# Order of the ScalarE and VectorE work in the recurrences, one turned group in another bank, and z ahead of the portions, in a fused gated-attention kernel

## The chip, the core and the metric

The kernel runs on one core of a Trainium2 chip. The metric is device microseconds of one execution, the median over runs. The kernel before takes 607.09 us (median of three runs, 606.45 to 607.91). The engines have short names: PE is TensorE, DVE is VectorE, ACT is ScalarE, POOL is GpSimd, SP is SyncE, which here only issues transfers.

## The reference

Three stages follow each other, for 4 batches of 768 tokens and 384 features, all in float32.

1. Gated linear attention, 8 heads of 48: `state = sigmoid(f) * state + k v`, `y = q state`, token by token.
2. A mixture of 4 attention experts of width 64: `softmax(scale * q k^T, causal) v wo` per expert, of which each token takes the two with the highest gate logits, weighted by their softmax.
3. `theta = x @ w_theta; z = (x cos theta, x sin theta); y = w_tok_r zr + w_tok_i zi; u = x + y; out = u + relu(u @ w_ch)`. The token mixing is a product of 768x768 with 768x384, twice a batch.

## The kernel before, in words

The tokens of a batch are cut into six chunks (or tiles) of 128, the heads into four pairs. Products that need float32 accuracy are made of three products of halves: a rounded part (`_h`, written by ACT) and the rest (`_l`, written by DVE, or by POOL for weights). Every engine has one queue, worked off in the order in which the code writes it, and the engines wait for each other by counting semaphores. So a line that waits also holds whatever is written behind it. `it` is the batch.

**Gates.** The gate logits of a batch go through five steps, in place in the tile `gate`: DVE clamps (`clamp_gates`, L804), ACT takes exp (`exp_gates`, L502) and ln(1+x) (`log_gates`, L507), DVE sums along the tokens (`scan`, L808), ACT writes exp(-sum) to `next_decay` together with a copy of the chunk sums (`shrink_pair`, L525) and exp(sum) in place (`grow_pair`, L531). POOL multiplies q by the first and k by the second (`scale`, L432). In batch 0 this goes by three parts of the tokens (`shrink_first`, `grow_first`, `scan_first`, `scale_first_q`, `scale_first_k`), with DVE scaling; in the others by pair, during the batch before. SP may load the gates of pair p of batch b+1 only when k of pair p of batch b is scaled (L346), since both use the same part of `gate`. `worst_sum` (DVE) takes the largest chunk sum and `worst_over_rows` (POOL, an all-reduce over the partitions) the largest over the rows; the flag `steep` that DVE makes of it decides on a slow path that the data never take, and DVE and ACT read it from memory at the end of each recurrence.

**Recurrence** (six chunks). PE makes masked scores, turns k (`turn_k`, L1223), adds the increments of the state and the outputs; DVE masks the scores (L935) and carries the state (L951, L955); ACT copies the turned k (`kTs`, L636) and the outputs (`xn`, L639). The code of the gates of the next batch is written between these.

**Ring.** PE turns xn to xT (L1382), then makes V with the gate logits of the experts (`wvg`) and q and k of the experts (`wqk`) through a ring of banks. DVE copies V, computes the routing (L1019 to L1039) and writes `qk_l` (L1058); ACT writes `xT_h` (L700) and `qk_h` (L704).

**Jobs.** Six jobs j of expert attention: scores (L1299), maxima on DVE (L1049), exp on ACT (L677), transposes of the probabilities in groups of at most four tiles (L1327), their copies (L1069 DVE, L713 ACT), the product with V into bank 7 (L1354). The turned groups use banks 4, 5 and 6 in turn: group g waits until group g-3 is copied. Every second job, `portions` (DVE, L1075 to L1079) makes the weight of each token for each expert, PE turns it (L1337), ACT copies it (L721) and DVE multiplies (`weigh_outputs`, L1091). At job 7 DVE clamps the gates of batch it+2, and PE begins the next batch's scores.

**Weights.** ACT and POOL split `wo`, its product with `w_theta` and `w_ch` into halves in the jobs of batch 0. The token weights are split in the jobs of batch 3 and later.

**Mixing.** Per batch six z tiles (`z_hi`, `z_lo`) times the token weights (`mix`), then the channel product. It begins inside the last jobs of batch 3, at job 6.

Of the kernel before, what the change touches and what calls it, by code (L numbers as in the profile page):

```python
# [22 lines left out]
P = 128  # L23
# [11 lines left out]
PART = 4  # L35
# [81 lines left out]
NG = len(GROUPS)  # L117

# [56 lines left out]
def build(nc, fT, qT, kT, vT, v, wq, wk, wv, w_gate, wo, woT, w_theta, w_tok, w_ch, out):  # L175
    with ExitStack() as ctx:
# [80 lines left out]
        worst_of_all = s1("worst_of_all", [P, 1])  # L257
        steep = s1("steep", [P, 1], I32)
# [146 lines left out]
        def _(pool):  # L405
# [41 lines left out]

            worst_over_rows(0)
# [33 lines left out]
            for tile in range(2 * TOKENS_FIRST):  # L482
                if tile >= 2 and tile % 2 == 0:
                    pool.wait_ge(spread_done, upto(B - 1, len(TILES), tile // 2))
                token_weights(tile)
# [15 lines left out]
        def _(act):  # L501
# [67 lines left out]

            def split_outputs(b):  # L570

                nc.scalar.copy(OT_h[:, :, :], OT[:, b:b + 1, :].rearrange("p b (a t) -> p (b a) t", a=2)).then_inc(oh, 1)
# [55 lines left out]
            for it in range(B):  # L628

                def recurrence_copies():  # L630
                    for c in range(NT):
                        if c < NT - 1:
# [3 lines left out]
                            nc.scalar.copy(kTs[:, c % 2, :], ps(7)).then_inc(kt_copied, 1)  # L636
                        if c >= 1:
                            act.wait_ge(y_done, upto(it, NT, c))
                            nc.scalar.copy(xn[:, c - 1, :], ps(4 + (c - 1) % 2)[:, 0:D]).then_inc(x_copied, 1)  # L639
                        if it < 1:  # L640
                            if c == 1:
                                shrink_first(2)
                                grow_first(2)
                            elif c == 3:
# [5 lines left out]
                            elif c in (4, 5):  # L650
                                exp_gates(it + 1, range(2 * c - 8, 2 * c - 6))
                        elif it < B - 1:
                            if c in (0, 1):
                                log_gates(it + 1, range(2 * c, 2 * c + 2))
# [25 lines left out]
                for n in [*range(RING_X), *range(FIRST_QK, RING)]:  # L680
                    if n == FIRST_QK:
# [7 lines left out]
                        if it < 1:  # L689
                            log_gates(it + 1)  # L690
                        if it < B - 1:
                            grow(it + 1, 0)
                            grow(it + 1, 1)
# [15 lines left out]
                def copy_turned(m):  # L709
                    for r in range(2):  # L710
                        g = group(m, r, PART)
                        act.wait_ge(pt_done, upto(it, NG, g + 1))
                        nc.scalar.copy(probT[:, m % 2, r, PART * P:WIDE], ps(4 + g % 3)[:, 0:WIDE - PART * P]  # L713
                                       ).then_inc(pt_copied[1], 1)

                def copy_portion(tp):
# [4 lines left out]
                    nc.scalar.copy(portion[:, :, :, :].rearrange("p w a t -> p (w a t)"), ps(4 + g % 3)  # L721
                                   ).then_inc(pt_copied[1], 1)

                for j in range(JOBS + 2):
# [8 lines left out]
                    if it < B - 1:  # L733
                        if j == (3 if it < 1 else 1):
                            shrink_pair(it + 1, 3)
                        elif j == (4 if it < 1 else 2):
                            grow_pair(it + 1, 3)
                    if it < 1:
                        if j == 1:
                            shrink_pair(1, 2)  # L740
                        elif j == 2:
                            grow_pair(1, 2)
                        elif j == 5:
                            act.wait_ge(w_in[2], 16)
                            hi(wx_h[:, :, 0:D], staged(W_O, 768, 2), w_hi)
                        elif j == 6:
                            hi(wx_h[:, :, D:2 * D], staged(W_OTH, 768, 2), w_hi)
                        elif j == 7:
                            act.wait_ge(w_in[4], 16)
                            hi(wch_h[:, :, :], staged(W_CH, 1152), w_hi)  # L750
                    if j == JOBS + 1 and it < B - 2:
                        exp_gates(it + 2)
                    if it > B - 2:
                        if j < 2 * TOKENS_FIRST:
                            token_weights(j)
                        if j == JOBS + 1:
                            split_outputs(0)

# [35 lines left out]
        def _(dve):  # L794
# [134 lines left out]
            for it in range(B):  # L929
# [11 lines left out]
                for c in range(NT - 1):  # L941
# [17 lines left out]
                    if it < 1:  # L959
# [559 lines left out]
```

## Time and profile before

| | |
|---|---|
| median of the runs | 607.09 us |
| the profiled execution | 607.17 us |
| its span, first to last instruction | 605.5 us |
| PE busy | 565.9 us, 93% |
| DVE, ACT, POOL busy | 377.0, 300.8, 128.0 us |
| recurrence, ring, jobs of batch 1 | 108 to 128, 128 to 155, 155 to 187 us |
| mixing, four batches | from 352 us on |
| mean granted PE clock | 0.997 of full speed |

Times in the rows are from the start of the span. A row of a timeline gives start, busy time, engine, line, operation, what it writes and reads, the count, and in brackets the idle time of that engine just before with what ended it. "issue" is time for which the profile shows no releaser.

### The profile page before, as it was taken

What the parts mean: (1) busy time and instruction counts of PE and PEld (TensorE: products, weight loads), DVE (VectorE), ACT (ScalarE), POOL (GpSimd) and SP (SyncE); (2) the same over time, 40 slices, a digit from 0 to 9 for tenths busy, and PEclk for the clock granted to TensorE, in tenths of its full rate; (3) what the DMA queues carried; (4) which work ended last, traced back from release to release, by engine and by line L of the source; (5) the groups of instructions that cost most, each with busy time, mean ns of one, the idle gap of its engine ahead of it and who ended that gap; (6) DMA issues with size and microseconds to landing.
All of it is one profiled execution on the core that took longest, in us unless ns stands there. A gap on an engine that the chain in (4) does not pass through costs nothing.

```text
span 605.5 us, 13205 instructions
## 1 busy us (share of the span) xinstructions
PE 565.9 (93%) x5532; PEld 522.5 (86%) x5532; DVE 377.0 (62%) x695; ACT 300.8 (50%) x623; POOL 128.0 (21%) x87
## 2 busy tenths in 40 slices
PE   0979899989999999999999989999999999999997
PEld 0779788889778897889997779999999999999997
DVE  3977877768677687766477748756244533454324
ACT  5658577644767356743377727513341334124311
POOL 1003431402330004400023216602220132013110
PEclk9999999999999999999999989999999999999999
DMA  8938111043110070000710000001000100010002
GB/s 289 318 108 289 37 44 28 2 160 130 54 54 2 15 276 1 1 1 4 260 55 2 1 1 2 0 15 66 0 1 1 70 9 1 1 53 28 0 1 79
DMA packets 17966, 37.19 MB, mean 61 GB/s; under 512 B 2160, under 2 KB 10608, under 8 KB 17392
## 3 DMA queue, kind: packets, MB, share of 16 engines
q1 hardware_dynamic: 17904, 36.32, 17.3%
q8 instruction: 44, 0.72, 0.5%
q14 instruction: 18, 0.15, 0.1%
HBM read 31.46 MB, written 4.72 MB: 60 GB/s over the span
## 4 chain that ended last, share of the span: by engine, by line
PE 75%; DVE 11%; ACT 9%; issue 3%; DMA 1%; SPq 0%; DVEq 0%; ACTq 0%
PE bank L1162 17%; PE bank L1163 16%; PE bank L1164 16%; PE bank L1327 5%; PE bank L1299 5%; PE bank L1354 4%; ACT prob L677 3%; PE bank L1180 3%; DVE nmax L1049 3%; PE bank L1260 2%; PE bank L1256 2%; PE bank L1444 1%; PE bank L1241 1%; PE bank L1227 1%; DMA gate<-fT 1%
## 5 line engine op out<-in xcount | busy, mean ns | idle before, releaser
L1162 PE MATMUL bank<-z_h,wt_h 128*128 128x384 f32 x288 | 98.3, 341 | 1.8 <-DVE z_l L889 1.8
L1163 PE MATMUL bank<-z_l,wt_h 128*128 128x384 f32 x288 | 98.1, 340 | 0.0
L1164 PE MATMUL bank<-z_h,wt_l 128*128 128x384 f32 x288 | 97.2, 338 | 0.0
L677 ACT ACTIVATE prob<-bank,nmax 128x384 f32<-128x384 f32 (+5 forms) x96 | 59.9, 630 | 26.9 <-DVE nmax L1049 26.7
L1049 DVE TENSOR_REDUCE nmax<-bank 128x1 f32<-128x384 f32 (+5 forms) x96 | 55.0, 618 | 20.9 <-PE bank L1305 14.6
L496 POOL TENSOR_TENSOR trig<-trig,x 128x768 f32<-128x768 f32 x18 | 33.6, 1865 | 151.9 <-ACT trig L597 92.6
L904 DVE TENSOR_SCALAR turns<-bank 128x384 int32<-128x384 f32 x22 | 12.2, 556 | 72.9 <-PE bank L1164 72.9
L1162 PEld LDWEIGHTS bank<-z_h,wt_h 128*128 128x128 f32 x288 | 54.4, 189 | 2.5 <-issue 2.2
L1163 PEld LDWEIGHTS bank<-z_l,wt_h 128*128 128x128 f32 x288 | 54.6, 189 | 0.0
L1164 PEld LDWEIGHTS bank<-z_h,wt_l 128*128 128x128 f32 x288 | 54.5, 189 | 0.0
L780 ACT CAST uT_h<-bank 128x384 fp32r<-128x384 f32 x24 | 11.5, 478 | 81.0 <-PE bank L1444 81.0
L1327 PE MATMUL bank<-ident,prob 128*128 128x128 f32 x336 | 46.0, 279 | 5.7 <-ACT portion L721 3.2
L1327 PEld LDWEIGHTS bank<-ident,prob 128*128 128x128 f32 x336 | 36.2, 141 | 14.1 <-ACT portion L721 5.1
L1354 PE MATMUL bank<-probT,Vm 128*64 128x128 f32 x672 | 42.0, 276 | 0.0
L1354 PEld LDWEIGHTS bank<-probT,Vm 128*64 128x64 f32 x672 | 36.2, 137 | 4.0 <-issue 4.0
L935 DVE TENSOR_TENSOR probT<-bank,keep 128x1024 f32<-128x1024 f32 x24 | 29.0, 1218 | 13.9 <-PE bank L1180 12.4
L589 ACT COPY x<-bank 128x384 f32<-128x384 f32 x24 | 11.6, 481 | 49.7 <-PE bank L1164 44.8
L1260 PE MATMUL bank<-V,probT 128*64 128x48 f32 x768 | 35.8, 219 | 0.0
L1162 PE MATMUL bank<-xT_h,wqk_h 128*128 128x384 f32 x96 | 32.9, 343 | 0.0
L1260 PEld LDWEIGHTS bank<-V,probT 128*64 128x64 f32 x768 | 31.9, 138 | 0.7 <-DVE probT L935 0.5
L1163 PE MATMUL bank<-xT_l,wqk_h 128*128 128x384 f32 x96 | 32.4, 338 | 0.0
L1164 PE MATMUL bank<-xT_h,wqk_l 128*128 128x384 f32 x96 | 32.4, 337 | 0.0
(177 smaller groups left out, 1391.8 us busy)
## 6 DMA issues: line engine op xcount, KB each, us to landing
V<-v SPq DMA_DIRECT2D x4, 1152.0 KB, 10.0
gate<-fT SPq DMA_DIRECT2D x12, 384.0 KB, 3.1
q<-qT SPq DMA_DIRECT2D x12, 384.0 KB, 6.1
k<-kT SPq DMA_DIRECT2D x12, 384.0 KB, 6.6
wt_raw<-w_tok SPq DMA_DIRECT2D x6, 768.0 KB, 8.0
out<-x SPq DMA_DIRECT2D x24, 192.0 KB, 1.9
gate<-fT SPq DMA_DIRECT2D x3, 512.0 KB, 4.9
q<-qT SPq DMA_DIRECT2D x3, 512.0 KB, 10.3
```

The lines of the kernel that those rows point to most:

```text
L496: nc.gpsimd.tensor_tensor(trig[:, s % 2, :, :], trig[:, s % 2, :, :], x2[:, s:s + 1, :].broadcast_to([P, 2, D]), ALU.mult).then_inc(z_made, 1)
L677: nc.scalar.activation(prob[:, m % 2, r, at], bank[r][:, at], ACT.Exp, bias=nmax[:, m, k:k + 1], accum_out=den[:, m // 2, which, e:e + 1]) ...
L935: nc.vector.tensor_tensor(Am[:, c % 2, :, :], bank[c % 2][:, :].rearrange("p (h t) -> p h t", h=H), keep[:, None, :].broadcast_to([P, H, P ...
L1049: nc.vector.tensor_reduce(nmax[:, m, k:k + 1], bank[r][:, columns_of(m, which)], X, ALU.max, negate=True).then_inc(max_done, 1)
L1162: nc.tensor.matmul(o, a_h, b_h, start=start, stop=False)
L1163: nc.tensor.matmul(o, a_h, b_l, start=False, stop=False)
L1164: return nc.tensor.matmul(o, a_l, b_h, start=False, stop=stop)
L1180: mm = nc.tensor.matmul(bank[c % 2][:, slot(h):slot(h) + P], k[r:r + 64, h // 2, at], q[r:r + 64, h // 2, at], start=True, stop=True)
L1260: mm = nc.tensor.matmul(ps(4 + c % 2)[own, h * HD:(h + 1) * HD], Am[:, c % 2, slot(h) // P, own], V[:, c, h * HD:(h + 1) * HD], start=(c = ...
L1299: mm = nc.tensor.matmul(bank[r][:, lo_:hi_], x[rows, a, queries], y[rows, 2 + a, keys], start=fresh_bank and n == 0, stop=False, skip_grou ...
L1327: mm = nc.tensor.transpose(ps(4 + g % 3)[:, (c - n) * P:(c - n + 1) * P], prob[:, m % 2, r, c * P:(c + 1) * P], ident[:, :])
L1354: mm = nc.tensor.matmul(ps(7)[64 * r:64 * r + 64, at], Vm[:, s, e * ED:(e + 1) * ED], probT[:, m % 2, r, n * P:(n + 1) * P], start=s == 0, ...
```

## The change

In the recurrences: in batch 0, ACT's growths of part 2 move behind the kTs copy of chunk 2, DVE scales k of part 2 right after q, and the clamps and exponentials of the next batch's gates move to chunk 4 and 5 and behind the ring's xT. In batches 1 and 2, ACT takes one pair's logarithm in each of the first four chunks, and the growth of pair 0 moves from the ring into chunks 4 and 5. In the jobs of batch 0, ACT shrinks or grows one pair in every job; the late weights move to the ring of batch 1. DVE's scan of pair 3 in batch 0 moves behind the maxima of job 0. POOL runs one all-reduce at its start, of which nothing uses the result. Turned group 3 goes to bank 7. In batch 3, DVE writes z_l of tile 0 in front of the portions of job 6, and token weight 5 moves to job 7.

```diff
+def turn_bank(g):
+    return 7 if g == 3 else 4 + g % 3
...
@@ gpsimd
+            nc.gpsimd.partition_all_reduce(warm[:, :], halfpi[:, :], P, bass.bass_isa.ReduceOp.max).then_inc(consts, 1)
             worst_over_rows(0)
...
             for tile in range(2 * TOKENS_FIRST):
+                if tile == 2 * TOKENS_FIRST - 1:
+                    pool.wait_ge(ol, 2)
                 token_weights(tile)
@@ scalar
+            def late_weights():
+                act.wait_ge(w_in[2], 16)
+                act.wait_ge(w_in[4], 16)
+                act.wait_ge(wth_copied, 1)
+                hi(wx_h[:, :, 0:D], staged(W_O, 768, 2), w_hi)
+                hi(wx_h[:, :, D:2 * D], staged(W_OTH, 768, 2), w_hi)
+                hi(wch_h[:, :, :], staged(W_CH, 1152), w_hi)
...  recurrence_copies, for c in range(NT), behind the copy to kTs
+                        if it < 1 and c == 2:
+                            shrink_first(2)
+                            grow_first(2)
...  behind the copy to xn
-                            if c == 1:
-                                shrink_first(2)
-                                grow_first(2)
-                            elif c in (4, 5):
-                                exp_gates(it + 1, range(2 * c - 8, 2 * c - 6))
+                            elif c == NT - 1:
+                                exp_gates(1, (0, 1))
                         elif it < B - 1:
-                            if c in (0, 1):
-                                log_gates(it + 1, range(2 * c, 2 * c + 2))
+                            if c < PAIRS:
+                                log_gates(it + 1, range(c, c + 1))
+                            elif c == NT - 2:
+                                shrink_pair(it + 1, 0)
+                            else:
+                                grow_pair(it + 1, 0)
...  ring, n == FIRST_QK
                         if it < 1:
-                            log_gates(it + 1)
-                        if it < B - 1:
-                            grow(it + 1, 0)
+                            exp_gates(1, (2, 3))
+                            log_gates(1)
+                            grow(1, 0)
+                        elif it < B - 1:
+                            if it == 1:
+                                late_weights()
                             grow(it + 1, 1)
...  jobs
-                    if it < B - 1:
-                        if j == (3 if it < 1 else 1):
-                            shrink_pair(it + 1, 3)
-                        elif j == (4 if it < 1 else 2):
-                            grow_pair(it + 1, 3)
-                    if it < 1:
-                        (j 1, 2: shrink_pair(1, 2), grow_pair(1, 2); j 5, 6, 7: hi of wx_h, wx_h, wch_h)
+                    if it < 1 and 1 <= j <= JOBS:
+                        (shrink_pair if j % 2 == 1 else grow_pair)(1, (j + 1) // 2)
+                    elif 1 <= it < B - 1 and j == 1:
+                        shrink_pair(it + 1, 3)
+                    elif 1 <= it < B - 1 and j == 2:
+                        grow_pair(it + 1, 3)
                     if it > B - 2:
-                        if j < 2 * TOKENS_FIRST:
+                        if j < 2 * TOKENS_FIRST - 1:
                             token_weights(j)
                         if j == JOBS + 1:
                             split_outputs(0)
+                            token_weights(2 * TOKENS_FIRST - 1)
@@ vector
...  recurrence of batch 0, behind the state of chunk c
                         elif c == 1:
                             scale_first_q(2)
                             worst_sum(0)
-                        elif c == 2:
                             scale_first_k(2)
-                        elif c in (3, 4):
-                            clamp_gates(1, 2 * c - 6)
-                            clamp_gates(1, 2 * c - 5)
+                        elif c == NT - 2:
+                            clamp_gates(1, 0)
+                            clamp_gates(1, 1)
...  behind the last xT_l
+                if it < 1:
+                    clamp_gates(1, 2)
+                    clamp_gates(1, 3)
...  ring, behind qk_l of tile n (in batch 0 both scans stood here, at n 1 and 3)
                     if n == FIRST_JOB:
                         row_max(0)
+                        if it < 1:
+                            scan(1, 3)
...
+                    if it < 1 and n == 1:
+                        scan(1, 2)
+                    elif 1 <= it < B - 1 and n == 3:
+                        scan(it + 1, 3)
...  jobs
-                    if j == 4 and it < B - 1:
+                    if j == (JOBS if it < 1 else 4) and it < B - 1:
                         worst_sum(it + 1)
...
+                    if it > B - 2 and j == JOBS:
+                        z_lo(0, 0)
                     if j >= 2 and j % 2 == 0:
                         portions((j - 2) // 2)
-                        if j == JOBS:
-                            z_lo(0, 0)
@@ tensor, turn_probs (ps(4 + g % 3) is ps(turn_bank(g)) here and in all copies)
-                        if g >= 3:
-                            pe.wait_ge(pt_copied[turned_by(g - 3)], copies(it, g - 3))
+                        if g >= 4:
+                            before = g - 3 if g != 6 else 0
+                            pe.wait_ge(pt_copied[turned_by(before)], copies(it, before))
...  weigh_values
+                    if m < 1:
+                        pe.wait_ge(pt_copied[turned_by(3)], copies(it, 3))
```

## Rows read from the trace of the kernel before

**Rows 1.** The page, busy time and share of the span, PE.

```profile
PE 565.9 (93%) x5532; PEld 522.5 (86%) x5532; DVE 377.0 (62%) x695; ACT 300.8 (50%) x623; POOL 128.0 (21%) x87
```
**Rows 2.** Waits of PE by line: total us, times, longest.

```profile
PE bank L1227 <- ACT kTs L636: 2.7, 3, 1.0
...
PE bank L1327 <- DVE probT L1069: 2.5, 4, 0.6
```
**Rows 3.** Timeline of PE in the recurrence of batch 0.

```profile
31.52 0.66 PE L1227 MATMUL bank<-ident,k 128*128 128x128 f32 x4 [0.91 <-ACT kTs L636]
...
35.31 1.16 PE L1180 MATMUL bank<-q,k 64*128 64x128 f32 x16 [0.94 <-DVE k L833]
...
43.92 0.39 PE L1256 MATMUL bank<-S,q 128*64 128x96 f32 x4 [1.37 <-issue]
```
**Rows 4.** Timeline of DVE there.

```profile
41.53 1.22 DVE L935 TENSOR_TENSOR probT<-bank,keep 128x1024 f32<-128x1024 f32 x1 [1.55 <-issue]
```
**Rows 5.** Timeline of POOL there and in the ring.

```profile
37.50 0.38 POOL L429 PARTITION_ALL_REDUCE worst_of_all<-worst  x1 [33.33 <-issue]
...
46.34 1.82 POOL L446 TENSOR_TENSOR wvg_l<-prob,wvg_h 128x768 fp32r<-128x768 f32 x1 [8.47 <-issue]
...
48.30 3.51 POOL L446 TENSOR_TENSOR wqk_l<-OT,wqk_h 128x1536 fp32r<-128x1536 f32 x1
```
**Rows 6.** DVE and PE in the ring of batch 0, and DVE's clamps by line.

```profile
46.95 2.88 DVE L889 TENSOR_TENSOR xT_l<-bank,xT_h 128x384 fp32r<-128x384 f32 x6 [2.07 <-ACT xT_h L700]
...
53.49 1.75 DVE L812 TENSOR_TENSOR_SCAN gate<-fresh,gate 128x768 f32<-128x768 f32 x1
...
71.98 0.50 PE L1299 MATMUL bank<-qk_h 64*128 64x512 f32 x2 [1.07 <-DVE qk_l L1058]
...
L806 DVE TENSOR_SCALAR gate<-gate,floor 128x768 f32<-128x768 f32 x12 | 6.7, 613 | 0.0
```
**Rows 7.** End of batch 0: ACT, POOL, the gates' transfer, DVE, PE.

```profile
102.91 0.84 ACT L568 CAST wx_h<-OT 128x768 fp32r<-128x768 f32 x1
...
94.05 1.81 POOL L443 TENSOR_TENSOR k<-k,gate 128x768 f32<-128x768 f32 x1 [3.50 <-ACT gate L534]
...
gate<-fT SPq DMA_DIRECT2D x12, 384.0 KB, 3.1
...
105.52 0.76 DVE L1091 TENSOR_TENSOR OT<-bank,portion 128x256 f32<-128x256 f32 x2 [1.49 <-PE bank L1354]
...
106.88 0.66 PE L1227 MATMUL bank<-ident,k 128*128 128x128 f32 x4
```
**Rows 8.** Timelines of ACT and PE in batch 1's recurrence.

```profile
108.83 1.28 ACT L510 ACT_TABLE_LOAD   x1
...
110.13 1.58 ACT L510 ACTIVATE gate<-gate 128x768 f32<-128x768 f32 x2
...
112.23 0.66 PE L1227 MATMUL bank<-ident,k 128*128 128x128 f32 x4 [1.01 <-ACT kTs L636]
```
**Rows 9.** PE ahead of the fifth xT tile in batches 1 and 3.

```profile
131.10 1.01 PE L1382 MATMUL bank<-ident,xn 128*128 128x128 f32 x6 [1.49 <-DVE xT_l L889]
...
294.61 1.01 PE L1382 MATMUL bank<-ident,xn 128*128 128x128 f32 x6 [0.18 <-DVE xT_l L889]
```
**Rows 10.** DVE, POOL and PE at job 6 of batch 3, and granted clock by window.

```profile
348.64 1.55 DVE L1075 TENSOR_SCALAR share<-den 128x8 f32<-128x8 f32 x1
...
348.33 1.82 POOL L470 TENSOR_TENSOR wt_l<-wt_raw,wt_h 128x768 fp32r<-128x768 f32 x1 [4.51 <-ACT wt_h L584]
...
352.16 0.41 PE L1162 MATMUL bank<-z_h,wt_h 128*128 128x384 f32 x1 [1.82 <-DVE z_l L889]
...
355.88 0.60 PE L1337 MATMUL bank<-ident,spread 128*128 128x128 f32 x4
...
350.00:354.00 4.00, 2.18 (x10) 1.97 (x9) 1.95 (x4) 0.48 (x1) 0.16 (x1) 0.81 0.00 0
...
366.00:370.00 4.00, 4.00 (x25) 4.00 (x24) 2.75 (x4) 3.97 (x7) 1.55 (x1) 1.00 0.00 0
```

More of the change, by code:

```diff
@@ L257, in build @@
         worst_of_all = s1("worst_of_all", [P, 1])
+        warm = s1("warm", [P, 1])
         steep = s1("steep", [P, 1], I32)
@@ L640, in recurrence_copies @@
                         if it < 1:
-                            if c == 1:
-                                shrink_first(2)
-                                grow_first(2)
-                            elif c == 3:
+                            if c == 3:
                                 act.wait_ge(w_in[0], 32)
@@ L712, in copy_turned @@
                         act.wait_ge(pt_done, upto(it, NG, g + 1))
-                        nc.scalar.copy(probT[:, m % 2, r, PART * P:WIDE], ps(4 + g % 3)[:, 0:WIDE - PART * P]
+                        nc.scalar.copy(probT[:, m % 2, r, PART * P:WIDE], ps(turn_bank(g))[:, 0:WIDE - PART * P]
                                        ).then_inc(pt_copied[1], 1)
@@ L720, in copy_portion @@
                         act.wait_ge(ot_done, upto(it, NT, NT + 2 * tp))
-                    nc.scalar.copy(portion[:, :, :, :].rearrange("p w a t -> p (w a t)"), ps(4 + g % 3)
+                    nc.scalar.copy(portion[:, :, :, :].rearrange("p w a t -> p (w a t)"), ps(turn_bank(g))
                                    ).then_inc(pt_copied[1], 1)
@@ L732, in _ @@
                         copy_turned(j - 1)
-                    if it < B - 1:
-                        if j == (3 if it < 1 else 1):
-                            shrink_pair(it + 1, 3)
-                        elif j == (4 if it < 1 else 2):
-                            grow_pair(it + 1, 3)
-                    if it < 1:
[L739 to L750, printed above, removed]
+                    if it < 1 and 1 <= j <= JOBS:
[4 more added lines that the diff above has]
+                        grow_pair(it + 1, 3)
                     if j == JOBS + 1 and it < B - 2:
@@ L1061, in _ @@
                                                    op1=ALU.subtract).then_inc(ring_free, 1)
-                    for p, last in ((2, 1), (3, 3)) if it < 1 else ((3, 3),):
-                        if n == last and it < B - 1:
-                            scan(it + 1, p)
+                    if it < 1 and n == 1:
+                        scan(1, 2)
+                    elif 1 <= it < B - 1 and n == 3:
+                        scan(it + 1, 3)
                 def copy_turned(m, r):
@@ L1068, in copy_turned @@
                     dve.wait_ge(pt_done, upto(it, NG, g + 1))
-                    nc.vector.tensor_copy(probT[:, m % 2, r, 0:PART * P], ps(4 + g % 3)).then_inc(pt_copied[0], 1)
+                    nc.vector.tensor_copy(probT[:, m % 2, r, 0:PART * P], ps(turn_bank(g))).then_inc(pt_copied[0], 1)
                 def portions(tp):
@@ L1112, in _ @@
                     if it > B - 2:
-                        if j == JOBS:
-                            z_lo(0, 0)
-                        elif j == JOBS + 1:
+                        if j == JOBS + 1:
                             split_outputs(0)
@@ L1323, in turn_probs @@
                         g = group(m, r, n)
-                        if g >= 3:
-                            pe.wait_ge(pt_copied[turned_by(g - 3)], copies(it, g - 3))
+                        if g >= 4:
+                            before = g - 3 if g != 6 else 0
+                            pe.wait_ge(pt_copied[turned_by(before)], copies(it, before))
                         for c in range(n, min(n + PART, KEYS)):
-                            mm = nc.tensor.transpose(ps(4 + g % 3)[:, (c - n) * P:(c - n + 1) * P],
+                            mm = nc.tensor.transpose(ps(turn_bank(g))[:, (c - n) * P:(c - n + 1) * P],
                                                      prob[:, m % 2, r, c * P:(c + 1) * P], ident[:, :])
@@ L1332, in turn_portions @@
                     g = group(2 * tp + 1, None, 0)
+                    assert g > 6
                     pe.wait_ge(spread_done, upto(it, len(TILES), tp + 1))
@@ L1336, in turn_portions @@
                         for a in range(2):
-                            mm = nc.tensor.transpose(ps(4 + g % 3)[:, (2 * w + a) * P:(2 * w + a + 1) * P],
+                            mm = nc.tensor.transpose(ps(turn_bank(g))[:, (2 * w + a) * P:(2 * w + a + 1) * P],
                                                      spread[:, w, 2 * a:2 * a + 2, :], ident[:, :])
```

## The prediction

> **What bounds the kernel now.** I read four views in this order. The busy times: TensorE (PE) is busy 566 of 605.5 us [rows 1], so a change can pay only where PE stands idle or runs slowly. PE's waits by line: apart from the first weights' arrival, which is not touched, the idle time is small change, repeated per batch: a stall before the transposes of xT (step 7), 2.7 us on copies of kTs, 2.5 us before the fourth turned group of the first job [rows 2]. Then the timelines of each engine around every such stall, and last the granted clock, which is 1.00 everywhere but from 352 to 356 us.
>
> **Method.** I replay each changed stretch with the durations of the rows and say how much earlier (minus) or later (plus) PE passes a point than before. Times are in the frame of the kernel before; what comes earlier in the program shifts both sides alike. A stall taken off PE counts in full only if the next thing PE needs is ready; I name that thing each time.
>
> **1. Recurrence of batch 0: -2.4 us.** PE waits three times: 0.91 us for the copy kTs of chunk 2, which stands on ScalarE (ACT) behind the growths of part 2; 0.94 us for k scaled by VectorE (DVE); 1.37 us for the last state [rows 3]. The new order puts the kTs copy ahead of the growths: turn_k(3) goes to 30.6. k is scaled right after q, from 31.8 to 33.0, instead of 33.95: scores(4) start at 33.4, when outputs(2) end. DVE loses two clamps (1.1 us) ahead of reading the steep flag, so S of chunk 3 is there at 37.5, the flag is written at 37.6, its read takes 1.55 us [rows 4], the last mask (1.22 us) runs from 39.1, Su and S follow by 41.4. PE starts outputs(5) at 41.5, not 43.92. What is late next is that same chain: PE still idles some 0.7 us there. What can eat this gain is GpSimd (POOL): V's tiles need wvg_l, which is ready at 48.3, just as PE got there [rows 5]. Its start at 46.34 came 8.5 us after the all-reduce, which itself was recorded 5.7 us after its input (31.78). If these gaps are fixed after the time the all-reduce is asked for, nothing moves and the gain is 0.1. The added all-reduce runs at about 4 us, when POOL is free, and nothing else of POOL stands between it and the real one: I take it that the real one then comes at 32, the next operation is possible from 40.5, and wvg_l starts with the state of chunk 4, at 41.5. Range -2.5 to -0.1.
> The Trainium skill (GPSIMD Engine Reference, Instruction dispatch) says that the first call of a freshly loaded POOL kernel pays about 6 us of code load; the gap of 5.7 us agrees. By it the warm call moves this load to the start of the program.
>
> **2. Ring of batch 0: -0.5 us.** Two clamps (0.61 us, 0.55 apart) now stand behind the last xT_l (end 49.83) and ahead of the copies of V. The exponentials of pairs 2 and 3 (1.58 us as a pair, like the logarithms) follow, then the table load of 1.28 us, so the first logarithm is there at 54.15 and scan 0 starts at 54.2 instead of 53.49 [rows 6, 8]: the routing and the first four qk_l are 0.65 late, and so are the first scores. But scan 3 (1.75 us) now stands behind the maxima of the first job, no longer ahead of them. These are 0.9 earlier, the exponentials of job 0 too, qk_l of the last tile ends at 71.4, and the piece of PE that waited for it starts at 71.5 instead of 71.98. ACT drops one pair's growth there (1.6 us) for the two exponentials. Upper bound +1.5: a clamp that meets wqk_l (3.5 us on POOL [rows 5]) waits for its end, and by the old times of POOL, less 2.4 us only in what is in front, that costs DVE 2 us. That such waits exist is shown by a tensor_scalar of 8 elements that took 1.55 us and ended with POOL's wt_l [rows 10]. By the times that I take, wqk_l ends at 47.0 and the clamp begins at 47.4.
> The skill (SBUF — State Buffer, Who interferes with whom) has it that a VectorE tensor_scalar in a 2-port mode and GpSimd block each other for a whole instruction; the trace agrees (those 1.55 us). By this rule the ring is -0.5 or +1.5, according to the 0.4 us between the two times.
>
> **3. Fourth turned group in bank 7: 4 x -0.6 = -2.4 us.** It no longer waits for DVE's copy of group 0; the rows have 2.5 us in four times [rows 2]. Next needed is exp_done of job 1 (75.2 against 74.8 plus a piece of scores), then the maxima of job 2, for which DVE waited on PE anyway. Bank 7 was last read before job 1's scores, and the values that use it wait for this group's copy, a whole job later. Range -1.2 to -2.5: ACT's growth of 0.85 us just behind can hold half of it.
>
> **4. End of batch 0: +3.9 us.** This is the step that speaks against the change. Pair 3's growth moves from job 4 to job 6, behind the copy that ends at 102.95, where wx_h stood [rows 7]. So gate grows by 103.75 and POOL scales k of pair 3 (1.81 us) until 105.6; before, it started that at 94.05. SyncE loads the gates of pair 3 of batch 2 only after it: 3.1 us to landing, 108.75. DVE clamps them in front of the last weighing of outputs, in the same queue: clamp until 109.35, the two products (0.76) until 110.1; before, they started at 105.52. PE needs these for turn_k(0) of batch 1: 110.15 instead of 106.88. DVE's first mask (1.22) then ends at 111.3, and outputs(0), which followed turn_k at 107.47, starts at 111.3: +3.9. Bounds: 0 (the transfer lands before 105) and +5.5 (POOL and DVE collide in scaling and clamps: twice 0.8).
>
> **5. Clock after that idle: +0.8 us.** PE idles 3.3 us there. After the idle of 1.82 us at 352 the granted clock of the next 4 us was 0.81 [rows 10], and work of 2.1 us took 3.7. Between nothing (after 1.49 us at 131 it stayed 1.00) and those 1.6 I take the middle, as DVE sets the pace of that stretch.
>
> **6. Waits for kTs: -2.0 us.** The table load of 1.28 and two logarithms (1.58) stand between two kTs copies in batches 1 and 2; PE waited 1.01 [rows 8] and 0.8 (2.7 in three [rows 2], less 0.91 and 1.01). With one logarithm the copy is 0.75 earlier: -0.7 in batch 2. In batch 1 ACT works on while PE stands still (step 4), so both waits, 0.3 for the first copy and 1.01, go: -1.3. The other logarithms stand where ACT idles 1.2 to 2.8 us a chunk.
>
> **7. Table load ahead of xT_h: 2 x -1.2 = -2.4 us.** In batches 1 and 2, where the last function ahead of the branch is the logarithm, 1.28 us of load stand at L700 and PE waits 1.49; in batch 3, without it, 0.18 [rows 9]. Now a growth comes ahead of the branch; its own load and exponential (2.3 us) lie in chunk 4, behind the copy of chunk 3 and well ahead of that of chunk 4. ACT's late weights of batch 1 (2.85 us) take the place of a growth of 1.7 and the idle time before the scan; POOL's parts of them are done 25 us before they are needed. Worst case -1.0 for both (another load stays), best -2.6.
>
> **8. z_l in front of the portions: -3.5 us.** z_l waited behind share, reciprocal and spread, 2.4 us with the collision of [rows 10]; token weight 5, which caused it, is moved too. z_l now ends at 349.5, PE's transposes end at 350.3, and mix starts then, not at 352.16: -1.85. Spread (until 350.7) is ready before mix ends. Without the idle the clock stays up, and the twelve products that took 3.7 us (352.16 to 355.88) take 2.1, at the pace of 25 in 4 us after 366: -1.6. Range -1.8 to -3.5.
>
> **Sum.** -2.4 - 0.5 - 2.4 + 3.9 + 0.8 - 2.0 - 2.4 - 3.5 = -8.5 us. The profiled execution took 607.17 us in all (span 605.5), the median of three is 607.09, so they are one number: 607.2 - 8.5 = 598.7 us.
>
> **Rivals.**
> A, the gates of batch 2 are not late: landing by 105.5, or clamped after the weighing. For: 3.1 us is a median. Against: the order on every queue. Steps 4 and 5 go and step 6 shrinks to -1.7: 594.3 us.
> B, POOL is as late as before: wvg_l starts near 46.3, PE waits for it, and the clamps of step 2 run into wqk_l: -0.1 and +1.5 for -2.4 and -0.5, together 603.0 us.
> C, slower: the clock stays low. One mechanism, at the start of batch 1: after 3.3 us without PE work the clock falls, and the small products of the recurrence do not raise it. At 0.81 the products of [rows 10] took 1.76 times as long, so 1 us of old work costs 0.76 more. It has to hold for 11 us of work to eat 8.5 us; over the whole recurrence and ring of batch 1 (46 us) it would cost up to 35. With the 20 us until the next dense stretch it gives 613 us. Against: at 352 it was back after 4 us.
> D, the small gains do not add (3 and 7 are taken back by ACT in the same job or ring): half of 3, 6 and 7, so +3.4: 602.1 us.
>
> **Chances.** Forecast 0.52, A 0.14, B 0.14, D 0.14, C 0.06. All but C are faster by more than 0.2% (1.2 us, about what a measurement of this kernel can tell); I leave 0.04 for no change where B and D come together with the collisions of step 4. So faster 0.90, same 0.04, slower 0.06. Range: A below and B above belong in it, 594.0 to 603.5; C is left out.
>
> **What would show it.** Step 1: outputs(5) of batch 0 starts 2.4 us earlier and wvg_l's gap is gone. Step 2: the first clamp behind xT_l takes 0.6 us, or over 2. Step 3: no wait at L1327 for DVE's probT. Step 4: between the batches DVE idles some 4 us before a clamp that waits for gate's DMA, and PE waits about 3.3 us at the first turn_k of batch 1. Step 5: PEclk under 1 there. Step 7: no table load at L700. Step 8: no wait of PE for z_l, PEclk 1.00 near 350. If step 4 doesn't show, the time is near 594; if the clock is low for more than 10 us in batch 1, the sign is wrong.

## The result

The changed kernel takes 601.34 us (median of four runs, 598.96 to 602.51) against 607.5 us of the kernel before in the same rounds. The medians differ by 6.2 us. The ratio is 0.9895, with a 95% interval of 0.9857 to 0.9933, which by itself gives 6.4 us less, between 4.1 and 8.7. The forecast was 8.5 less. The profiled execution is the slowest of the four, 602.51 us with a span of 600.8 and a mean granted clock of 0.991 (before: 0.997); the fastest had 0.996. The clock is thus one part of the spread.

The waits of PE by line, in the profile after (total us, times, longest):

```profile
PE bank L1320 <- DVE qk_l L1078: 3.2, 5, 1.9
...
PE bank L1248 <- DVE OT L1112: 3.1, 1, 3.1
...
PE bank L1349 <- ACT portion L748: 3.0, 8, 0.4
...
PE bank L1277 <- issue: 1.4, 4, 0.7
...
PE bank L1407 <- DVE xT_l L905: 0.9, 4, 0.4
...
PE bank L1360 <- DVE spread L1100: 0.3, 1, 0.3
```

The waits of [rows 2] for kTs and for probT are gone, the one for xT_l (3.6 us before) is down to 0.9. Two are new or grown: 1.88 us for qk_l in the ring of batch 0 and 3.05 us for OT at the end of batch 0. The next fences follow these two through the engines. First the ring of batch 0, timelines of POOL, DVE and PE and the granted clock (the number before the last two of a window's row):

```profile
14.12 0.41 POOL L456 PARTITION_ALL_REDUCE warm<-halfpi  x1 [9.95 <-issue]
...
32.96 1.13 POOL L437 PARTITION_ALL_REDUCE worst_of_all<-worst  x1 [18.42 <-DVE worst L854]
...
43.97 1.82 POOL L454 TENSOR_TENSOR wvg_l<-prob,wvg_h 128x768 fp32r<-128x768 f32 x1 [9.88 <-issue]
...
45.93 3.50 POOL L454 TENSOR_TENSOR wqk_l<-OT,wqk_h 128x1536 fp32r<-128x1536 f32 x1
```
```profile
48.09 2.29 DVE L822 TENSOR_SCALAR gate<-gate,floor 128x768 f32<-128x768 f32 x2
...
53.65 1.76 DVE L828 TENSOR_TENSOR_SCAN gate<-fresh,gate 128x768 f32<-128x768 f32 x1 [1.74 <-ACT gate L521]
```
```profile
65.02 0.59 PE L1320 MATMUL bank<-qk_h 64*128 64x384 f32 x2 [1.88 <-DVE qk_l L1078]
```
```profile
65.20:68.50 3.30, 3.30 (x21) 2.19 (x22) 2.06 (x5) 1.23 (x4) 0.00 (x0) 0.50 0.00 0
```

POOL's wqk_l is in flight from 45.93 to 49.43. DVE's two clamps need 1.15 us elsewhere and 2.29 here: the first one waits for POOL. Scan 0, which in [rows 6] came without a wait, waits 1.74 us for the logarithm behind them, PE waits 1.88 us for the first scores, and then works at half its clock until 68.5.

Then the end of batch 0, timelines of ACT, POOL, DVE and PE, and the clock:

```profile
102.86 0.85 ACT L545 ACTIVATE gate<-gate 128x768 f32<-128x768 f32 x1
```
```profile
103.85 2.25 POOL L451 TENSOR_TENSOR k<-k,gate 128x768 f32<-128x768 f32 x1 [1.48 <-ACT gate L545]
```
```profile
101.05 1.34 DVE L1096 TENSOR_SCALAR share<-den 128x8 f32<-128x8 f32 x1
...
109.25 0.62 DVE L822 TENSOR_SCALAR gate<-gate,floor 128x768 f32<-128x768 f32 x1 [2.74 <-DMA gate<-fT]
...
109.78 0.75 DVE L1112 TENSOR_TENSOR OT<-bank,portion 128x256 f32<-128x256 f32 x2
```
```profile
110.68 1.09 PE L1248 MATMUL bank<-ident,k 128*128 128x128 f32 x4 [3.05 <-DVE OT L1112]
```
```profile
109.60:116.30 6.70, 5.62 (x63) 4.88 (x64) 3.75 (x6) 4.25 (x6) 0.38 (x1) 0.50 0.01 2
```

This is the chain of step 4 link by link: growth of pair 3 until 103.7, POOL's scaling until 106.1, the transfer, DVE idle 2.74 us "<-DMA gate<-fT", the clamp, the products, and PE after 3.05 us of nothing. The scaling took 2.25 us in place of 1.81, beside DVE's other clamps. The clock is 0.50 from 109.6 to 116.3, and PE works for 5.6 us of that. In [rows 7] DVE began the same products at 105.52 and PE its transposes at 106.88 without a wait.

Last, three places where the change gained: the last state of the first recurrence, the xT transposes of batch 1, and z_l:

```profile
42.25 0.39 PE L1277 MATMUL bank<-S,q 128*64 128x96 f32 x4 [0.73 <-issue]
```
```profile
134.54 1.01 PE L1407 MATMUL bank<-ident,xn 128*128 128x128 f32 x6 [0.18 <-DVE xT_l L905]
```
```profile
347.57 0.95 DVE L905 TENSOR_TENSOR z_l<-x,z_h 128x768 fp32r<-128x768 f32 x1
...
348.43 0.16 DVE L1096 TENSOR_SCALAR share<-den 128x8 f32<-128x8 f32 x1
```

The wait of 1.37 [rows 3] is 0.73, that of 1.49 [rows 9] is 0.18. z_l ends at 348.5, share behind it takes 0.16 us instead of 1.55 [rows 10], and PE shows no wait for z_l and a clock of 1.00 there.

How far PE is ahead of (-) or behind (+) the kernel before at the start of the same work, and what each stretch gave against its step:

| PE starts | before | after | difference | stretch | forecast |
|---|---|---|---|---|---|
| first scores, batch 0 | 20.89 | 21.84 | +0.95 | +0.95 (start) | 0 |
| xT of batch 0 | 45.65 | 43.98 | -1.67 | -2.62 (step 1) | -2.4 |
| first turned group, batch 0 | 73.01 | 73.91 | +0.90 | +2.57 (step 2) | -0.5 |
| scores of job 2, batch 0 | 75.54 | 75.58 | +0.04 | -0.86 (step 3) | -0.6 |
| outputs(0) of batch 1 | 107.47 | 111.71 | +4.24 | +4.20 (step 4) | +3.9 |
| turn_k(2) of batch 1 | 112.23 | 116.98 | +4.75 | +0.51 (steps 5, 6) | -0.5 |
| V of batch 1 | 132.03 | 135.47 | +3.44 | -1.31 (step 7) | -1.2 |
| scores of job 2, batch 1 | 158.11 | 160.72 | +2.61 | -0.83 (step 3) | -0.6 |
| turn_k(2) of batch 2 | 194.00 | 195.92 | +1.92 | -0.69 (step 6) | -0.7 |
| V of batch 2 | 213.81 | 214.40 | +0.59 | -1.33 (step 7) | -1.2 |
| scores of job 2, batches 2 and 3 | 323.51 | 322.44 | -1.07 | -1.66 (step 3) | -1.2 |
| portions of job 7, batch 3 | 355.88 | 351.21 | -4.67 | -3.60 (step 8) | -3.5 |

### The profile page after: what moved, and what is told of

Its sections match the earlier page's. It is cut to its first block, busy times and chain, and to the rows that moved or that the text cites. A ratio compares the mean times of both kernels' runs of the same rounds, so it can differ in the third digit from the quotient of the medians.

```text
span 600.8 us, 13212 instructions
## 1 busy us (share of the span) xinstructions
PE 568.6 (95%) x5532; PEld 524.8 (87%) x5532; DVE 379.5 (63%) x695; ACT 300.7 (50%) x623; POOL 131.5 (22%) x88
## 4 chain that ended last, share of the span: by engine, by line
PE 81%; DVE 8%; ACT 6%; DMA 2%; issue 2%; SPq 1%; POOL 0%; DVEq 0%; ACTq 0%; POOLq 0%
PE bank L1183 17%; PE bank L1184 16%; PE bank L1185 16%; PE bank L1349 6%; PE bank L1320 5%; PE bank L1379 4%; PE bank L1201 3%; ACT prob L701 3%; PE bank L1281 3%; PE bank L1277 2%; PE bank L1248 2%; PE bank L1262 2%; DVE nmax L1067 2%; PE bank L1469 1%; DMA OT<-w_theta 1%
```

## The experiments

**1. Growths of batch 1's pairs in the order of before.** The version called early_growth:

```diff
                             log_gates(1)
                             grow(1, 0)
+                            grow(1, 1)
...
-                    if it < 1 and 1 <= j <= JOBS:
-                        (shrink_pair if j % 2 == 1 else grow_pair)(1, (j + 1) // 2)
+                    if it < 1 and 1 <= j <= 4:
+                        (shrink_pair if j % 2 == 1 else grow_pair)(1, (j + 1) // 2 + 1)
...
-                    if j == (JOBS if it < 1 else 4) and it < B - 1:
+                    if j == 4 and it < B - 1:
```

> The changed kernel with the growths of batch 1's pairs in the order of before: pairs 0 and 1 in the ring, pair 2 in jobs 1 and 2, pair 3 in jobs 3 and 4 (and the worst sum at job 4). Theory: the late growth of pair 3 delays the gates of batch 2, DVE's clamp and PE. Then PE's wait of 3.05 us at the first turn_k of batch 1, its wait of 0.3 for spread and the low clock behind (about 1.5) go, and about 1 us of the waits for kTs comes back less than before: 3.9 us less than the changed kernel's 601.3, so 597.4 us. Rival: PE's wait there has another cause (the chain of the last values), it stays, and the time is 601 within the noise. Second rival: the growth back in the ring delays the routing's exponential and the first scores by 1 us or more: above 598.5.

594.23 us (593.46 to 595.23), ratio to the kernel before 0.9792 (0.976 to 0.9823): 7.1 less than the changed kernel. The wait for OT is gone, and so is every wait for kTs. Between the portions of job 7 and turn_k(2) of batch 1, PE gains 5.8 us on the changed kernel (from -2.74 to -8.55): 3.05 of wait, 0.3 in the scores ahead of it (1.95 us in the changed kernel, whose last k POOL had ready at 106.1, and 1.61 here), and 2.3 in work that ran at half clock. This end of batch 0 cost more than steps 4 and 5 said, because I had put 0.8 us on the low clock. The other 2.7 us by which the two profiles differ are the start (1.1; PE's first scores at 20.75, not 21.84), 0.3 at the portions, and 1.4 in the ring, where a wait of 2.00 us is not followed by a low clock here. So of the 7.1 us between the medians some 6 belong to the edit, and the rest is what differs from one execution to the next.

**2. All four clamps in chunk 4 of the recurrence.** The version early_clamps:

```diff
                         elif c == NT - 2:
-                            clamp_gates(1, 0)
-                            clamp_gates(1, 1)
+                            for p in range(PAIRS):
+                                clamp_gates(1, p)
...
-                if it < 1:
-                    clamp_gates(1, 2)
-                    clamp_gates(1, 3)
```

> The changed kernel with all four clamps of batch 1's gates in chunk 4 of batch 0's recurrence, none behind the last xT_l. Theory: the clamp behind xT_l waits for POOL's wqk_l, and with what follows makes PE wait 1.9 us for the first scores, after which its clock falls. DVE has 2 us idle behind chunk 4's clamps, so nothing else moves: the clamps end before xT_l begins, scan 0 starts about 1.5 us earlier, PE's wait of 1.9 us shrinks under 0.4 and the clock stays up in the ring: 3.1 us less than 601.3, so 598.2 us. Rival: the exponentials of pairs 2 and 3 on ACT with the table load set the start of scan 0, not the clamp: the wait stays over 1 us and the time is over 600.

598.9 us (597.69 to 599.43), ratio 0.9859 (0.9829 to 0.989); 2.4 less than the changed kernel. Its wait of 1.88 us is gone, the four waits of PE for qk_l are 1.3 us in all, and scan 0 starts without one. DVE's clamps now meet POOL's wvg_l, and take 3.79 us instead of 2.2; PE pays 0.5 for that (0.9 us of wait for xT_l in place of 0.4):

```profile
PE bank L1317 <- DVE qk_l L1075: 1.3, 4, 0.3
...
PE bank L1245 <- DVE OT L1109: 3.1, 1, 3.1
```
```profile
40.66 3.79 DVE L822 TENSOR_SCALAR gate<-gate,floor 128x768 f32<-128x768 f32 x4
```

**3. Both edits together,** version both.

> Both of these edits. Theory: they are independent (one is paid in the ring, one at the end of batch 0), so 3.9 and 3.1 add: 594.3 us. Rival: the second growth in the ring on ACT takes back 1 us of it: 595.3 us or more.

592.81 us (592.5 to 594.06), ratio 0.9764 (0.9735 to 0.9793). It is 8.5 us below the changed kernel and 14.7 below the kernel before. The second edit is worth only 1.4 on top of the first, not 3.1: by the profiles it gains 1.9 in the ring and loses 0.5 ahead of it, at the wait for xT_l, and early_growth had no low clock in the ring that could go.

**4. What holds the clamp: POOL makes wqk_l later.** On early_growth:

```diff
+            pool.wait_ge(clamped, gates(1, PAIRS))
             lo(wqk_l[:, :, :], staged(W_QK, 1536), wqk_h[:, :, :], wqk_lo)
```

> The early_growth version (594.2 us), in which POOL makes wqk_l only when the clamp of pair 3 of batch 1 is done. In early_growth the two clamps behind the last xT_l took 2.10 us, in recurrence 1.14, and PE waited 2.0 us for the first scores. Theory: the 0.95 us more is the wait for wqk_l, in flight on POOL. Then the two clamps take 1.15 us, scan 0 starts 0.95 earlier, PE's wait falls to about 1.0 (two clamps, two exponentials and the table load remain ahead of scan 0), and wqk_l is done before q and k need it: 593.3 us. Rival: the clamps were slow for another reason: they stay at 2.1 and the time at 594.2 or more.

593.08 us (592.76 to 593.61), ratio 0.9773 (0.9756 to 0.9789). The clamps and PE's wait, in early_growth and then here:

```profile
46.99 2.10 DVE L823 TENSOR_SCALAR gate<-gate,floor 128x768 f32<-128x768 f32 x2
```
```profile
64.04 0.44 PE L1321 MATMUL bank<-qk_h 64*128 64x384 f32 x2 [2.00 <-DVE qk_l L1079]
```
```profile
47.05 1.14 DVE L824 TENSOR_SCALAR gate<-gate,floor 128x768 f32<-128x768 f32 x2
```
```profile
63.15 0.44 PE L1322 MATMUL bank<-qk_h 64*128 64x384 f32 x2 [1.04 <-DVE qk_l L1080]
```

2.10 us became 1.14, and 2.00 became 1.04: the clamp did wait for wqk_l, and PE paid all of it. The other 1.0 us of wait is the late clamps' own work with the exponentials and the table load, of which step 2 had 0.6.

**5. When POOL can go on.** On both, POOL waits for the state of chunk 3 instead of chunk 4 ahead of wvg_l (`pool.wait_ge(s_ready, NT - 2)`), version pool_early:

> Both edits, and POOL waits for the state of chunk 3, not of chunk 4, ahead of wvg_l. In the changed kernel the all-reduce was recorded until 34.1, the state of chunk 4 was there at 42.15 and wvg_l started at 43.97. Theory 1 (the gap is fixed after the all-reduce, 8.5 to 9.9 us): wvg_l starts at 42.6 to 44.0 as now. Theory 2 (a start about 2 us after the wait is met): the state of chunk 3 is there at 38.3, wvg_l starts near 40.2. In time: 594.3 us in either case by my account, as PE gets to V when wvg_l is ready either way; by theory 2 POOL's reads may slow DVE's last states, up to 1 us more.

592.72 us (592.1 to 592.95), ratio 0.9762 (0.9732 to 0.9791), level with both. Timelines of POOL, pool_early first, then both:

```profile
32.05 1.13 POOL L437 PARTITION_ALL_REDUCE worst_of_all<-worst  x1 [16.25 <-DVE worst L855]
...
42.37 2.17 POOL L454 TENSOR_TENSOR wvg_l<-prob,wvg_h 128x768 fp32r<-128x768 f32 x1 [9.19 <-issue]
```
```profile
33.31 1.13 POOL L437 PARTITION_ALL_REDUCE worst_of_all<-worst  x1 [17.96 <-DVE worst L855]
...
43.95 1.83 POOL L454 TENSOR_TENSOR wvg_l<-prob,wvg_h 128x768 fp32r<-128x768 f32 x1 [9.51 <-issue]
```

The operation starts 9.2 us after the all-reduce's end here and 9.5 there, though the wait was met a chunk (some 4 us) earlier; by theory 2 it would have started near 40. So most of the gap hangs on the all-reduce, not on the wait. In all versions with the added all-reduce it is 9.2 to 9.9.

**6. Without the all-reduce at the start,** version no_warm, on both:

> The same version (592.8 us) without the all-reduce at the start. Theory: the first all-reduce that runs carries about 6 us of code load, wherever it is. Then the real one is recorded 5.7 us or more behind its input, not 0.35, and what POOL does next comes about 9.5 us after it: wvg_l starts near 48, not 43.9, PE waits 2 us or more for it ahead of V, and the flag is read up to 1 us later: 595 to 597 us. Rival: the gap behind the all-reduce counts from when it was asked for, as in the kernel before (8.5 us after its record, 14.2 after its input): wvg_l starts near 46.5, and the cost is under 1 us: 593.5 us.

```profile
37.40 0.38 POOL L437 PARTITION_ALL_REDUCE worst_of_all<-worst  x1 [33.23 <-issue]
...
44.56 1.82 POOL L454 TENSOR_TENSOR wvg_l<-prob,wvg_h 128x768 fp32r<-128x768 f32 x1 [6.78 <-issue]
```
```profile
37.81 0.15 DVE L994 TENSOR_SCALAR steep<-worst_of_all 128x1 int32<-128x1 f32 x1 [0.77 <-POOL worst_of_all L437]
```

593.85 us (593.05 to 595.95), ratio 0.9794 (0.977 to 0.9818), 1.0 more than both; the intervals overlap, but the profile shows the mechanism. The all-reduce is recorded 5.9 us behind its input (31.5, not shown) instead of 0.2, DVE waits 0.77 us for it, and PE's longest wait at L1275 grows from 0.7 to 1.6. But POOL goes on after 6.8 us instead of 9.5. The rival was right: the added all-reduce takes 5.7 us away ahead of the real one, and 2.7 come back behind it. From its first scores to its first product for V, PE takes 0.6 us longer than in both, so that is what the added all-reduce is worth here.

The theory was wrong in a second point: the 6 us are not a cost of the first all-reduce alone. In the profiles of all versions, every `worst_over_rows` that comes behind other work of POOL, in batches 1 to 3 too, is recorded 5.7 to 6.6 us after its input and that work were done.

**7. Group 3 back in bank 4,** version bank3, on both (`return 4 + g % 3`, and its wait for group 0):

> The version with early growth and early clamps (592.8 us), with group 3 turned into bank 4 again, as before the change. Theory: PE waits 0.63 us for DVE's copy in each of the four batches, and only that comes back: 2.5 us more, 595.3 us. Rival: the waits come back but the next one (for ACT or DVE in the same job) shrinks by as much: 592.8 to 593.8 us.

596.12 us (595.87 to 600.36), ratio 0.9842 (0.9803 to 0.9881), 3.3 more. PE's four waits for probT return with 2.5 us. From the first turned group to the scores of job 2 it takes 2.53 us again, as in the kernel before, and not 1.68; of the 0.85 us next to nothing comes back in the same job, so 0.8 us a batch is lost. The waits of the products and of the weight loads (PEld):

```profile
PE bank L1346 <- DVE probT L1088: 2.5, 4, 0.6
```
```profile
PEld bank L1346 <- DVE probT L1088: 3.5, 4, 0.9
```

The weight loads, which run ahead of the products, stood still for the whole 3.3 to 3.5 us; the rows on the products alone, which I had used, show less.

**8. z_l and token weight 5,** on both. z_half puts z_lo behind the portions again; z_old also puts token weight 5 back to job 5 and takes POOL's wait for ol away.

> The same version (592.8 us) with z_l of tile 0 behind the portions again, but token weight 5 still at job 7. Theory: z_l then waits for share, reciprocal and spread without a collision with POOL, 1.05 us, and PE, which was 0.7 us behind z_l, waits about 0.4 us; the clock stays up: 593.2 us. Rival: the order alone was the cause of the old wait of 1.82 us: 596 us.

> The same version (592.8 us) with z_l behind the portions and token weight 5 at job 5, both as before the change. Theory: share waits for POOL's wt_l (1.55 us in place of 0.16), PE waits 1.8 us for z_l and its clock falls for about 3 us of work, which costs 1.6 more: 596.3 us. Rival: without the fall of the clock 594.6 us.

z_half 593.3 us (592.42 to 593.71; ratio 0.9769, 0.9752 to 0.9785), z_old 595.78 (594.61 to 596.15; ratio 0.9808, 0.9792 to 0.9824). Timelines of PE and DVE, z_half and then z_old, and z_old's clock behind the wait:

```profile
340.21 0.41 PE L1181 MATMUL bank<-z_h,wt_h 128*128 128x384 f32 x1 [0.44 <-DVE z_l L906]
```
```profile
342.61 0.41 PE L1178 MATMUL bank<-z_h,wt_h 128*128 128x384 f32 x1 [1.82 <-DVE z_l L903]
```
```profile
339.09 1.55 DVE L1091 TENSOR_SCALAR share<-den 128x8 f32<-128x8 f32 x1
```
```profile
342.60:346.60 4.00, 3.99 (x40) 3.79 (x42) 0.00 (x0) 1.18 (x2) 0.00 (x0) 1.00 0.01 4
```

Of the old wait of 1.82 us, 0.44 comes from the order alone and 1.4 from share waiting for POOL. The two together cost 3.0 us in the median, 2.1 in the profiles. The clock did not fall in z_old's profile.

**9. The clamp of pair 3 out of the way,** on the changed kernel, version late_clamp:

```diff
-                            for p in range(PAIRS):
+                            for p in range(PAIRS - (it < 1)):
                                 clamp_gates(it + 2, p)
...  behind mask(0)
+                elif it == 1:
+                    clamp_gates(2, 3)
...  ACT, job 7, and chunk 0 of batch 1
-                        exp_gates(it + 2)
+                        exp_gates(it + 2, range(PAIRS - (it < 1)))
+                            if it == 1 and c == 0:
+                                exp_gates(2, (3,))
```

> The changed kernel (601.3 us) with one move at the end of batch 0: the clamp of pair 3 of batch 2's gates stands behind the first mask of batch 1 on DVE, its exponential behind the first copy of kTs on ACT; the late growths stay. Theory: what stops PE is that the clamp, which waits for the transfer, stands in front of the last weighing of outputs. Then PE's wait of 3.05 us at turn_k(0) goes, although the gates land at the same time; a wait of 1.5 to 2 us for kTs of chunk 1 comes, as ACT waits for the clamp and then loads its table; the clock may still fall: 597.5 to 600 us. Rival: POOL's late scaling of k is what delays PE (the scores of heads 6 and 7 wait for it): then the wait stays 3 us.

596.97 us (595.74 to 598.39), ratio 0.9842 (0.981 to 0.9873), 4.4 less than the changed kernel. The wait for OT is gone; one for kTs has come. DVE and PE:

```profile
106.31 0.62 DVE L824 TENSOR_SCALAR gate<-gate,floor 128x768 f32<-128x768 f32 x1 [0.98 <-DMA gate<-fT]
```
```profile
110.50 0.66 PE L1252 MATMUL bank<-ident,k 128*128 128x128 f32 x4 [1.82 <-ACT kTs L656]
```

The growths are as late here as in the changed kernel, so it is the place of the clamp in DVE's queue that stopped PE, not the late scaling by itself. In the profiles the move is worth 3.5 us between the portions of job 7 and the xT of batch 1. The late growths still cost PE 2.3 us there against early_growth, of which 1.82 is the new wait for kTs. The two profiles differ elsewhere by 3 us, at the start and in the ring, where PE waited 1.5 us here and the clock stayed at 1.00; no edit of this version touches that.

**10. Only the recurrences of batches 1 and 2,** on the kernel before: one logarithm a chunk, growth of pair 0 in chunks 4 and 5. Version only_rec:

> The kernel before (607.5 us) with one part of the change: in batches 1 and 2, one logarithm a chunk and the growth of pair 0 in chunks 4 and 5. Theory: PE's waits for kTs in batches 1 and 2 fall by 0.7 each, and the table load at L700 goes, 1.2 each: 3.8 us less, 603.7 us. Rival: the table load comes back in front of xT_h, as copies need a table too: 606.1 us.

603.3 us (602.0 to 603.93), ratio 0.994 (0.9918 to 0.9962), 3.8 less. Waits of PE for kTs (2.7 before) and xT_l (3.6 before), and ACT's table load of batch 1, now in chunk 4:

```profile
PE bank L1232 <- ACT kTs L636: 1.2, 2, 0.9
...
PE bank L1387 <- DVE xT_l L894: 0.9, 4, 0.4
```
```profile
123.42 1.28 ACT L529 ACT_TABLE_LOAD   x1
```

In the profile PE gains 0.7 us in each of the two recurrences and 1.3 at each xT, 4.1 in all.

## Why the prediction was right, and where it was not

The time, its direction and the sum's form held; the sum was 2.3 us too good in the median and 3.8 in the profiled execution. Some of the agreement is luck: steps 2 and 5 came out worse than forecast by more than 4 us together, step 3 came out better, and what the low clock adds differs from one execution to the next.

- **Step 1** (-2.4): -2.6, with the chain of the recurrence as it was replayed. The all-reduce came at 32.96, 0.2 us behind its input, as assumed. Its bound of -0.1 was too cautious: without the added all-reduce (experiment 6) the recurrence is still 1.8 us shorter than in the kernel before. No run takes the new order of the kTs copy, the scaling and the clamps back singly.
- **Step 2** (-0.5) is the step that failed: +2.6. The failing link is "the next operation is possible from 40.5 and wvg_l starts at 41.5", taken from the gap of 8.5 us in [rows 5]. With the added all-reduce the gap is 9.9, wvg_l started at 43.97, and wqk_l stood in the clamp's way until 49.43. In the frame of the kernel before (0.95 less) the clamp began at 47.1, near the 47.4 of the forecast, and wqk_l ended at 48.5, not 47.0. The 0.4 us between the two times was no margin; I had the upper bound of +1.5 from this very collision and gave it too little. Experiment 4 shows the collision, at 1.0 us. The second miss is in the same step: its bound had no clock in it, and the low clock behind the wait cost 1.5 us more (from the first scores to the first turned group PE took 8.9 us, and 7.4 in every later version with scan 3 behind the maxima, none of which had a low clock there). That stretch took 8.1 us before, so moving scan 3 gave 0.8 of the 1.15 that it had in the forecast.
- **Step 3** (-2.4): -3.35 in the profile, 3.3 by experiment 7. The mechanism held, the term was mis-sized: 0.8 a batch, the wait of the weight loads, not the 0.63 of the products.
- **Step 4** (+3.9): +4.2. Experiments 1 and 9 show cause and place. The collision of share with POOL's scaling (1.34 us, the row at 101.05) was in the bounds and cost PE 0.3.
- **Step 5** (+0.8) was mis-sized: the clock was 0.50 from 109.6 to 116.3, and 1.00 from 116.4 on, which cost 2.3 us against experiment 1. The forecast rested on a wrong reading of [rows 10]: the 0.81 there is the mean of a stretch that begins 2.2 us before PE goes on at 352.16, and it is not the clock of the work behind the wait. That was 0.50, as in the changed kernel (kernel before, granted clock):

```profile
352.50:355.80 3.30, 3.30 (x12) 3.29 (x11) 0.00 (x0) 0.00 (x0) 0.00 (x0) 0.50 0.00 0
```

The factor of 1.76 that rival C puts beside 0.81 is thus the price of work at 0.50. Steps 5 and 6 in batch 1 together gave +0.5 instead of -0.5: 1.9 of the low clock fall behind outputs(0), and -1.4 is step 6, which had -1.3. By experiment 1 the end of batch 0 cost 5.8 us, where steps 4 and 5 had 4.7.
- **Steps 6 and 7** (-2.0 and -2.4): -0.7 in batch 2 and -1.3 twice; experiment 10 gives 3.8 in the median and 4.1 by the stretches of its profile, where 3.8 was expected. No table load was left ahead of xT_h, L700 of the kernel before.
- **Step 8** (-3.5): -3.6 in the profile, of which 2.1 is the earlier start of mix and 1.5 the clock, 0.50 before and 1.00 now. Experiment 8 gives 2.1 in the profiles, where the clock stayed up, and 3.0 in the median. So the forecast counted on the clock falling in the kernel before, which it does not do in every execution: in only_rec, whose code there is that of the kernel before, PE waited the same 1.82 us and the clock stayed at 1.00. In the experiments' rounds the kernel before took 605.4 to 606.6 us in the 8 executions with a mean clock of 1.000, and 606.8 to 608.9 in the 16 with 0.997; where the clock fell is known only of the profiled one. By experiment 8 three quarters of the wait was token weight 5, not the order.
- **The start** (+0.95) was in no step. PE's first products, which no edit touches, took 5.56 to 7.14 us over the profiles of all versions, and the first scores began at 20.4 to 22.7. Each of the twelve products takes 0.85 us at first and 0.49 later; what differs is when they double their pace, 3.3 us after the first in the kernel before and 5.9 in the changed one. That differs from one execution to the next by as much as a single term, and can be part of the 3.5 us between the four runs.

Of the rivals, B was half right (the clamps ran into wqk_l, but wvg_l did not hold PE), and A and C were wrong: the gates were late, and the clock was back 5.7 us after PE went on. D was wrong; every small gain came.

## What to carry over

When an edit moves work to a later place, follow every transfer that its end sets free to the queue in which the arrival is awaited: here one growth moved two jobs later stopped PE for 3 us through POOL, a transfer and a clamp, and moving one clamp took that away. Where two engines only just miss each other in a replay, and the miss is smaller than the spread of the gap that it rests on, price the collision in full; and price an idle time of PE near 2 us or more with the slow work behind it: where the clock fell, that cost 1.5 us behind waits of 1.82 and 1.88 us, and 2.3 behind one of 3.05. Read the clock of that work from a stretch that begins where the work does.

## What the runs showed of the hardware

- **An SBUF tensor_scalar that begins on DVE while a POOL tensor_tensor is in flight ends only behind it.** A pair of clamps took 1.14 us alone and 1.85 to 2.29 beside wqk_l; share of 8 elements took 0.16 alone and 1.55 beside wt_l, and ended with it. Four clamps beside wvg_l took 3.79 instead of 2.2. A clamp under way when POOL began took its 0.61 us, and POOL's scaling then 2.25 instead of 1.81.
- **POOL's all-reduce costs on both sides of itself.** Recorded as 0.4 to 1.1 us, the all-reduce of `worst_over_rows` came 5.7 to 6.6 us after its input and POOL's other work were done, every time and not only the first, but 0.2 us behind its input when another all-reduce was POOL's last operation. Where nothing else held POOL, its next operation came 6.4 to 9.9 us after it. The added one at the start was recorded at 14.12, though POOL had nothing else to do since 4.17.
- **The same idle time does not always lower the clock.** It was 0.50 behind 1.82 us of idle PE in the kernel before and 1.88 in the changed kernel; behind 1.82 us in z_old, only_rec and late_clamp, and 2.00 in early_growth, it stayed 1.00. Around the idle times of 3.05 us in the changed kernel and 3.1 in early_clamps it was 0.50 for 6.7 us. What decides near 2 us these runs do not show.
